# Moving the two halves of the key split behind the normalisations on GpSimd, in the attention stage of a fused kernel

## The reference, cut to what matters

```python
scores = scale * np.matmul(q, k.transpose(0, 1, 3, 2))
thresh = np.max(scores, axis=-1, keepdims=True) - tau
scores = np.where(scores >= thresh, scores, -1e9)
attn = np.exp(scores - max); attn = attn / (sum(attn) + 1e-9)
x = np.matmul(attn, v)            # per batch and head
x = moe(x)                        # each token through one of 8 experts
out = mixing(x)                   # theta, cos/sin, token mixing, channel mixing
```

## Time and profile before

| | |
|---|---|
| median of 3 runs | 891.58 us (891.46 to 895.08) |
| the profiled execution | 891.46 us |
| its span, first to last instruction | 889.5 us |
| TensorE busy | 798.9 us, 90% of the span |
| GpSimd busy | 521.3 us, 59% |
| VectorE busy | 448.0 us, 50% |
| ScalarE busy | 388.6 us, 44% |
| mean granted clock of TensorE | 0.965 |

### The profile page before, as it was taken

How to read it: one execution, slowest core, us unless ns; L and a number is a source line. 1 busy time by engine, 2 the same in 40 slices (tenths; PEclk the granted TensorE clock), 3 DMA queues, 4 the chain that set the end, 5 groups by cost and what they waited for, 6 DMA issues and landing times. The chain is left out here.

```text
span 889.5 us, 16449 instructions
## 1 busy us (share of the span) xinstructions
PE 798.9 (90%) x5056; PEld 678.7 (76%) x5057; DVE 448.0 (50%) x1044; ACT 388.6 (44%) x669; POOL 521.3 (59%) x461
## 2 busy tenths in 40 slices
PE   1889999999999723999999999998488999999998
PEld 1778878878877512788888888887377899898998
DVE  1868888888887363212222122222185756645622
ACT  1568878778777540221221212212275634524310
POOL 3556766776788803957699998998255703404100
PEclk9999999999999955999999999999799999999999
DMA  8978678678766053485655455581310110110101
GB/s 223 306 200 203 165 191 195 174 187 192 180 153 180 14 203 138 167 262 188 236 177 186 163 194 177 178 259 47 113 27 27 48 60 25 37 47 1 48 8 54
DMA packets 79397, 125.32 MB, mean 141 GB/s; under 512 B 26304, under 2 KB 39872, under 8 KB 79360
## 3 DMA queue, kind: packets, MB, share of 16 engines
q1 hardware_dynamic: 69232, 101.44, 39.8%
q0 software_dynamic: 3472, 11.28, 4.2%
q10 hardware_dynamic: 6656, 12.13, 4.2%
HBM read 70.55 MB, written 23.86 MB: 106 GB/s over the span
## 5 line engine op out<-in xcount | busy, mean ns | idle before, releaser
L324 POOL TENSOR_SCALAR p_ring<-p_ring,xs_nat 128x576 f32<-128x576 f32 x144 | 105.5, 747 | 80.0 <-DVE xs_nat L433 80.0
L514 PE MATMUL psum<-k_st,q_st 128*128 128x288 f32 x640 | 125.9, 326 | 24.6 <-DMA q_st<-q_split 18.2
L403 DVE TENSOR_REDUCE xs_nat<-psum 128x1 f32<-128x576 f32 x144 | 105.8, 749 | 47.4 <-PE psum L514 47.3
L514 PEld LDWEIGHTS psum<-k_st,q_st 128*128 128x128 f32 x640 | 94.4, 199 | 36.7 <-issue 21.6
L418 DVE SCALAR_TENSOR_TENSOR p_ring<-psum,xs_nat,e_ring 128x576 f32<-128x576 f32 x144 | 114.5, 811 | 15.6 <-PE psum L543 9.0
L1130 PE MATMUL psum<-w_split,x_hi 128*128 x352 | 116.9, 404 | 1.9 <-DVE x_lo L1210 1.9
L1057 POOL TENSOR_TENSOR w_split<-w_raw,w_split 128x1024 fp32r<-128x1024 f32 x48 | 115.3, 2403 | 4.0
L1151 PE MATMUL psum<-w_split,h_hi 128*128 x352 | 114.8, 397 | 3.2 <-DVE h_lo L1215 3.2
L626 ACT ACTIVATE e_ring<-psum,xs_nat 128x576 f32<-128x576 f32 x144 | 105.6, 749 | 20.6 <-DVE xs_nat L403 19.7
L644 ACT COPY p_t<-psum 128x512 f32<-128x512 f32 x144 | 84.4, 586 | 29.7 <-PE psum L532 26.6
L1337 POOL TENSOR_TENSOR stage<-g,xs_nat 128x512 f32<-128x512 f32 (+1 forms) x20 | 27.3, 1366 | 110.6 <-ACT xs_nat L1543 110.6
(11 more groups left out here) (185 smaller groups left out, 1560.5 us busy)
## 6 DMA issues: line engine op xcount, KB each, us to landing
w_raw<-w_dram SPq DMA_DIRECT2D x48, 512.0 KB, 3.5
k_st<-k_split SPq DMA_DIRECT2D x64, 320.0 KB, 5.4
q_st<-q_split SPq DMA_DIRECT2D x60, 144.0 KB, 2.6
xs_dram<-stage SPq DMA_DIRECT2D x23, 256.0 KB, 2.1
xs_nat<-xs_dram ACTq DMA_DIRECT2D x22, 256.0 KB, 3.1
ys_dram<-y_nat ACTq DMA_DIRECT2D x22, 256.0 KB, 2.5
k_nat<-k_t_dram SPq DMA_DIRECT2D x16, 320.0 KB, 4.2
q_nat<-q_t_dram SPq DMA_DIRECT2D x16, 288.0 KB, 4.8
```

The costliest lines, as they stand in the source:

```text
L324: pl.tensor_scalar(t, t, rsum[:, col:col + 1], 1.0, ALU.mult, ALU.mult).then_inc(s_norm, 1)
L403: dve.tensor_reduce(negmax[:, u % 3, 0:1], s_bank[u % 3][:, :, 0:HALF], AX.XY, ALU.max, negate=True).then_inc(s_max, 1)
L514: mm = pe.matmul(bank[:, x, 0:HALF], lhs, key[:, HALF * x:HALF * x + HALF], start=(j == 0), stop=(j == len(terms) - 1))
```

## The change

In GpSimd's list for a pair, `split(i + 1, m, 3)` and `split(i + 1, m, 4)`, the two passes over the keys of the pair two ahead, move. Part 3 now stands behind `norm(i, m, 6)` and `norm(i, m, 7)`, part 4 behind `norm(i, m, 8)` and ahead of `take_logits`. No instruction is added or removed, and the lists of the other engines stay as they are.

```diff
             if parts:
                 split(i + 1, m, 2)
-                split(i + 1, m, 3)
-                split(i + 1, m, 4)
             if here:
                 norm(i, m, 6)
                 norm(i, m, 7)
+            if parts:
+                split(i + 1, m, 3)
             piece(1)
             if here:
                 norm(i, m, 8)
+            if parts:
+                split(i + 1, m, 4)
             if past:
                 take_logits(i, m - 1) if m else take_logits(i - 1, 1)
             if ahead:
```

## The result

The changed kernel takes 907.91 us (median of 4 runs, 906.61 to 910.52), the kernel before in the same series 893.21 us. The ratio is 1.0168 with a 95% interval of 1.0132 to 1.0204: slower, by about 15 us. The forecast was 903.1 us, range 895.5 to 908.5. The reference of this series is 1.6 us above the 891.58 us that the forecast started from, so the loss itself was 15 us where 11.6 were forecast.

The account below looks back on a forecast made before the run. TensorE's list, busy 16.82 us a pair, was taken as the bound. A wait of 0.95 us in 11 pairs (10.5 us) plus 0.7 and 0.4 us in pairs 14 and 15 took 891.46 to 903.1 us, range 895.5 to 908.5.

Parts of the forecast that it names:

- Norm 6 gains little and norm 8 nothing: GpSimd's norms: norm 6 starts 0.48 us sooner; norm 8 ends at 148.57 against 148.37, still ahead of its consumer.
- The inverse, not part 2, releases norm 6; part 4 slips: GpSimd's list: norm 6 waits for VectorE's inverse until 145.70, so part 4 ends 3.87 us later, at 150.08.
- The four key copies take 7.9 us alone: SyncE's key copies: with no query copies ahead, the last lands 7.9 us after the first issue, at 158.1.
- The 5.0 us of the estimate: Key copies by the skill's DMA page: all land 5.0 us after the first issue, TensorE never waits, 891.5 us.
- The loop closes every pair and nothing is caught up: Attention's middle pairs: the period becomes 17.8 us against 16.82 in every pair, since TensorE has no gap to give.
- The term: TensorE's wait for late keys at a pair's first scores: 0.95 us a pair, bounds 0.45 to 1.35 us.
- 0.7 and 0.4 us on these two: Loss in pairs 14 and 15, where gaps from GpSimd's weight pieces were to swallow part of the 0.95 us wait.
- its upper bound: Largest loss forecast for the attention pairs: 1.35 us x 12.2 = 16.5 us, giving 908 us.
- Rival A: Key copies land before TensorE's scores need them, 7.0 us after first issue instead of 7.9: 891.5 us, chance 0.13.
- Rival B: Faster: TensorE takes norm 6 and its followers sooner, 0.48 us gained in each of 14 pairs: 884.8 us, chance 0.04.
- Rival C: Worse: SyncE's later loads slip past its waits or share the transfers, wait doubles to 1.9 us: 914 us, chance 0.05.

Follow-up runs that it names:

- the last kernel: Kernel before with 15 early transfers dealt out over pairs 0 to 9 and GpSimd's weight pieces spread over pairs 10 to 15: 880.44 us, ratio 0.9868.

## Why the prediction was right

- *Norm 6 gains little and norm 8 nothing.* Right: norm 6 starts 2.49 us behind `last_keys(0)` as reckoned, and no wait for a norm appears in the middle pairs.
- *The inverse, not part 2, releases norm 6; part 4 slips.* Right to 0.01 us: 6.88 us behind the start of `last_keys(0)` against 143.21 to 150.08 = 6.87.
- *The four key copies take 7.9 us alone.* 8.1 us. Halving the copies took the wait away and two queues did not speed them up, so it is the transfer that TensorE waits for, and its pace is not that of one queue (195 GB/s by one, 199 by two). The 5.0 us of the estimate under which TensorE would never wait did not come.
- *The loop closes every pair and nothing is caught up.* Right, and shown by part 4's ends at 6.18, 6.88 and 7.28 us, which gave pairs of 17.41, 18.00 and 18.44 us.
- *The size.* The term was 0.95 us a pair and measured 1.17 in the pair shown and 1.24 in the mean: 0.2 us more from the copies (8.1 for 7.9), 0.1 us more until TensorE reacts (0.2 for 0.1), 0.1 us less until SyncE issues (0.03 for 0.12). 13 pairs instead of 12.2 paid it, since pairs 14 and 15 swallowed nothing: from 77.54 to 294.71 twelve intervals of 18.1 us. The forecast had put 0.7 and 0.4 us on these two, and they measured 1.1 and 1.4. The start lost 0.4 us and the tail 0.9. Together 17.4 us in the trace where 11.6 were forecast, which is more than the 16.5 us of its upper bound. The median of the runs grew by 15 us and stands 0.6 us inside the range, the profiled execution (909.75 us) outside it: the mechanism held, but that the number fell into the range was in part luck.
- *Rival A* (the keys land in time) fell: 8.1 us, not 7.0. *Rival B* named a wait on norm 8 that does not exist in this order; one norm ahead of the key parts creates it. *Rival C* did not come: the store goes out on time.

What was only argued: that no order with both key parts behind the inverse can meet both deadlines. Three of the possible orders were run.

## What to carry to other kernels

When work is moved out of an engine's idle time, follow its result through the queue and the transfer to the engine that sets the pace: here 1.6 us of slack in a queue and 1.2 us at the landing covered 2.8 of a slip of 3.9 us, and what was left was paid in each of 13 pairs. List every deadline behind the moved work, not only the one that the change is about. And a jam in a queue isn't cleared by moving it one place on; dealing it out in portions that fit the queue's rests gave 5.8 us, half of the last kernel's 1.3%; the rest came with the spread weight pieces.

## What the runs showed of the hardware that I had not expected

Key copies over disjoint halves of the partitions, issued from two engines, landed no sooner together (8.7 us for four of 320 KB, with loads between them) than from one (8.1 us), and all transfers together moved 199 against 195 GB/s. The page "SBUF — State Buffer" of the Trainium skill, section "Door 1: the DMA port swizzle", gives each half its own 8 ports, by which alone the two streams could have run side by side. The same page's section "Can I just issue two DMAs to hit both halves?" says that they don't: both run on the same DMA engines and serialize, with 6% gained in its measurement. This case's traces agree with the second, though the two halves were only arranged by the order of issue and not forced to meet.
